# Row maxima of one main tile per head, taken for both heads together with 64-row products around the tails' products with v

## What is computed

```python
q_rot, k_rot = (rotate(q), rotate(k))
scores = scale * np.matmul(q_rot, k_rot.transpose(0, 1, 3, 2))
scores = scores - np.max(scores, axis=-1, keepdims=True)
attn = np.exp(scores)
attn = attn / (np.sum(attn, axis=-1, keepdims=True) + 1e-09)
attn_out = np.matmul(attn, v)                     # [4, 8, 576, 64], all float32
x = attn_out.transpose(0, 2, 1, 3).reshape(2304, 512)
h = x @ w_in                                      # [2304, 1024]
e = np.exp(h - h.max(-1, keepdims=True)); sm = e / (e.sum(-1, keepdims=True) + 1e-09)
solu = h * sm
ln = (solu - solu.mean(-1, keepdims=True)) / np.sqrt(solu.var(-1, keepdims=True) + 1e-06) * g_ln
out = ln @ w_out
```

## Time and profile before

| | us |
|---|---|
| median of 3 runs | 489.78 (489.76 to 490.06) |
| the profiled execution | 490.39 |
| its span, first to last instruction | 488.6 |
| PE busy | 479.5 |
| DVE busy | 362.6 |
| ACT busy | 255.4 |
| POOL busy | 179.0 |

### The profile page before, as it was taken

One profiled execution on the slowest core, in us unless ns is written; L12 is line 12 of the kernel. 1 busy time (PEld: TensorE's weight loads), 2 busy tenths in 40 slices (PEclk: granted clock), 3 DMA queues, 4 the chain that ended last, 5 costly groups with the idle time before them and its releaser, 6 DMA issues.

```text
span 488.6 us, 7547 instructions
## 1 busy us (share of the span) xinstructions
PE 479.5 (98%) x2499; PEld 402.5 (82%) x2499; DVE 362.6 (74%) x566; ACT 255.4 (52%) x383; POOL 179.0 (37%) x208
## 2 busy tenths in 40 slices
PE   7899999999999999999999999999999999999997
PEld 7677888888888888888888878888888888888885
DVE  6866877786787678677866446999998899888731
ACT  4666776777687777767777343133223222222221
POOL 6855164336435542643460012233343121122110
PEclk9999999999999999999999999999999999999999
DMA  8306454535454454545433112233333233322232
GB/s 282 95 15 171 129 166 99 171 133 162 120 147 147 117 175 125 170 99 162 138 94 97 26 46 34 48 67 85 82 70 79 36 68 68 81 55 59 61 73 89
DMA packets 101006, 50.57 MB, mean 104 GB/s; under 512 B 90280, under 2 KB 90280, under 8 KB 99048
## 3 DMA queue, kind: packets, MB, share of 16 engines
q1 hardware_dynamic: 100152, 50.00, 38.5%
q10 hardware_dynamic: 816, 0.10, 0.1%
HBM read 33.33 MB, written 4.79 MB: 78 GB/s over the span
## 4 chain that ended last, share of the span: by engine, by line
PE 92%; DMA 2%; DVE 2%; ACT 1%; POOL 1%; SPq 1%; issue 1%; POOLq 0%; DVEq 0%; ACTq 0%
PE ps L1017 24%; PE ps L1045 20%; PE ps L1031 20%; PE ps L984 17%; PE ps L955 8%; PE ps L999 4%; DMA X<-x_in 2%; POOL X L379 1%; DVE nm L735 1%; SPq L281 0%; ACT p_main L548 0%; DVE X L676 0%; DVE X L702 0%; ACT QK L504 0%; DVE X L681 0%
## 5 line engine op out<-in xcount | busy, mean ns | idle before, releaser
L735 DVE TENSOR_REDUCE nm<-ps 128x1 fp32r<-128x576 f32 x144 | 108.1, 755 | 56.8 <-PE ps L955 54.8
L1017 PE MATMUL ps<-p_main,V 128*128 128x288 f32 x512 | 145.4, 406 | 0.0
L548 ACT ACTIVATE p_main<-ps 128x576 f32<-128x576 f32 x128 | 83.2, 650 | 47.4 <-PE ps L984 45.8
L379 POOL TENSOR_TENSOR X<-X,rope 128x1152 f32<-128x1152 f32 x28 | 73.5, 2644 | 91.6 <-DVE w_lo L752 89.1
L1017 PEld LDWEIGHTS ps<-p_main,V 128*128 128x128 f32 x512 | 90.1, 190 | 13.7 <-ACT p_main L548 0.2
L984 PE MATMUL ps<-QK 128*128 128x288 f32 x320 | 95.8, 380 | 0.8 <-ACT p_main L548 0.5
L1031 PE MATMUL ps<-w_hi,KB 128*128 128x512 f32 x288 | 91.4, 390 | 0.0
L1045 PE MATMUL ps<-w_hi,QK 128*128 128x512 f32 x288 | 91.0, 389 | 0.0
L984 PEld LDWEIGHTS ps<-QK 128*128 128x128 f32 x320 | 57.6, 189 | 20.8 <-issue 5.7
L984 PE MATMUL ps<-KB 128*128 128x288 f32 x320 | 67.8, 293 | 0.0
L569 ACT ACTIVATE X<-ps,neg_max 128x1024 f32<-128x1024 f32 x18 | 20.1, 1119 | 83.1 <-DVE neg_max L773 83.1
(11 more groups left out here) (87 smaller groups left out, 574.6 us busy)
## 6 DMA issues: line engine op xcount, KB each, us to landing
X<-x_in SPq DMA_DIRECT2D x14, 1152.0 KB, 5.1
V<-oe SPq DMA_DIRECT2D x213, 32.0 KB, 1.9
V<-v_in SPq DMA_DIRECT2D x32, 160.0 KB, 2.8
out<-X SPq DMA_DIRECT2D x18, 256.0 KB, 2.3
w_raw<-w_in SPq DMA_DIRECT2D x16, 256.0 KB, 3.0
xT<-oe SPq DMA_DIRECT2D x16, 144.0 KB, 2.4
inv<-inv_rows SPq DMA_DIRECT2D x16, 144.0 KB, 3.0
xT<-oe SPq DMA_DIRECT2D x16, 128.0 KB, 2.3
```

Of the source, the lines that this page charges most:

```text
L379: nc.gpsimd.tensor_tensor(x, x, rope[:, :, :], ALU.mult).then_inc(done, 1)
L548: nc.scalar.activation(dst[:, :].rearrange("p (b c) -> p b c", b=2), score_ps[:, :, 0:HALF], ACT.Exp, scale=SCALE).then_inc(exp_done, 1)
L735: nc.vector.tensor_reduce(nm[g][:, at:at + 1], src[:, :, 0:HALF], AX_XY, ALU.max, negate=True)\
L1017: ins = nc.tensor.matmul(o_ps[a][:, half, 0:HALF], v, p[:, half * HALF:(half + 1) * HALF], start=(k == 0), stop=(k == 9))
```

## The change

For pairs `m` from 3 (`JOINT`) on, the fourth main tile of each head (tiles 3 and 8) is no longer made by two products over 128 rows. `joint_scores` makes both heads' tiles together: per half of the keys (288 of them) one product over a's 64 rows and one over b's 64 rows, into the two banks of the one place for maxima, from the high parts alone. The first half stands directly ahead of `weigh_tails` in step 5, the second directly behind it. DVE reduces each half to one value per query and head (`nm_half`), takes the smaller negated value of the two halves (`nm[2]`), and turns it (`turned[2]`). Step 6 has no maxima any more. The tail tile's maxima and b's first mains come a step earlier (`JOINT_ORDER`). `rows_of_a` and `rows_of_b` have one transfer less each, and the two rows of the joint tiles go out in `rows_of_both`, which stands in SP's list behind `load_x`. On DVE `w_low` moves from step 2 to step 1, and `add` stands between the two halves.

```diff
 STEPS = 9
+JOINT = 3
+
+JOINT_ORDER = (0, 1, 2, 4, 5, None, None, 6, 7)
...
+JOINT_MAXIMA = [((s,), (), ()) for s in range(5)] + [((5,), (), (6,)), ((), (), ()), ((7,), (), ()), ((8,), (), ())]
...
             def rows_of_a(m):
                 done = rows_early[m % 2]
                 sp.wait_ge(turned[0], m)
-                for j in range(BOTH):
+                for j in range(BOTH if m < JOINT else BOTH - 1):
                     row_part(m, 0, D, main_col(0, j), j, 4, done)
...
+            def rows_of_both(m):
+
+                sp.wait_ge(turned[2], m - JOINT + 1)
+                row_part(m, 2, D, main_col(0, BOTH - 1), 0, 4, rows_early[m % 2])
+                row_part(m, 2, 0, main_col(1, BOTH - 1), 1, 4, rows_late[m % 2])
...
                 if n + 3 < PAIRS:
                     load_x(n + 3)
+                if JOINT <= n + 1 < PAIRS:
+                    rows_of_both(n + 1)
                 if 1 <= n < PAIRS - 1:
                     inverse_out(n - 1)
...
+            def joint_max(m, k):
+
+                second = k % STEPS == BOTH + 2
+                nc.vector.tensor_reduce(nm_half[int(second)][:, :], max_slot(k)[0][:, :, 0:HALF], AX_X, ALU.max, negate=True)\
+                  .then_inc(max_taken, 1)
+                if second:
+                    dve.wait_ge(max_taken, k + 1)
...
+                    nc.vector.tensor_tensor(nm[2][:, 0:2], nm_half[0][:, :], nm_half[1][:, :], ALU.min)\
+                      .then_inc(halves_joined, 1)
+                    dve.wait_ge(halves_joined, m - JOINT + 1)
+                    nc.vector.transpose(nm_row[2][:, :], nm[2][:, :].bitcast(F32)).then_inc(turned[2], 1)
...
-                    if s == 2 and n >= 2:
+                    if s == 1 and n >= 2:
                         w_low(n - 2)
-                    if s == 5 and n + 2 < PAIRS:
-                        add(n + 2)
...
+            def joint_scores(m, k):
+
+                c, half = m % 2, k % STEPS - BOTH - 1
+                for a in range(2):
+                    at, keys = main_col(a, BOTH - 1), COLS[a] + half * HALF
+                    ins = nc.tensor.matmul(max_slot(k)[0][:, a, 0:HALF], QK[c][own(a), 0, at:at + P],
+                                           QK[c][own(a), 1, keys:keys + HALF], start=True, stop=True)
+                ins.then_inc(max_ready, 1)
```

More of the change, by code:

```diff
@@ L11 @@
 ACT = mybir.ActivationFunctionType
+AX_X = mybir.AxisListType.X
 AX_XY = mybir.AxisListType.XY
@@ L80, in attention_then_mlp @@
         rope = sb("rope", [P, 2, S])
-        nm = [sb(f"nm{g}", [P, TURN], F32R) for g in range(2)]
-        nm_row = [sb(f"nm_row{g}", [P, TURN]) for g in range(2)]
+        nm = [sb(f"nm{g}", [P, TURN], F32R) for g in range(3)]
+        nm_row = [sb(f"nm_row{g}", [P, TURN]) for g in range(3)]
+        nm_half = [sb(f"nm_half{h}", [P, 2]) for h in range(2)]
         tail_k = sb("tail_k", [P, S], F32R)
@@ L125, in attention_then_mlp @@
         max_taken = sem("max_taken")
-        turned = [sem(f"turned{g}") for g in range(2)]
+        turned = [sem(f"turned{g}") for g in range(3)]
+        joint_zero = sem("joint_zero")
+        halves_joined = sem("halves_joined")
         score_ready = sem("score_ready")
@@ L394, in set_tails @@
                 if m >= 2:
[L395 removed]
+                    pool.wait_ge(max_ready, STEPS * (m - 1) + tails_at(m - 1) + 1)
                     pool.wait_ge(tails_set, 3 * m - 3)
@@ L722, in low_queries, with row_max @@
                   .then_inc(low_q_done[a], 1)
-            def row_max(m, i):
-                k, g = STEPS * m + i, int(i > BOTH)
+            def joint_max(m, k):
[4 more added lines that the diff above has]
+                    dve.wait_ge(max_taken, k + 1)
+                    if m == JOINT:
+                        dve.wait_ge(joint_zero, 1)
+                    else:
+                        dve.wait_ge(turned[2], m - JOINT)
+                        dve.wait_ge(rows_early[(m - 1) % 2], early(m - 1))
+                        dve.wait_ge(rows_late[(m - 1) % 2], uses(m - 1) * LATE * 16)
+                    nc.vector.tensor_tensor(nm[2][:, 0:2], nm_half[0][:, :], nm_half[1][:, :], ALU.min)\
+                      .then_inc(halves_joined, 1)
+                    dve.wait_ge(halves_joined, m - JOINT + 1)
+                    nc.vector.transpose(nm_row[2][:, :], nm[2][:, :].bitcast(F32)).then_inc(turned[2], 1)
+            def row_max(m, place):
+                k, i = STEPS * m + place, tile_at(m, place)
                 dve.wait_ge(max_ready, k + 1)
+                if i is None:
+                    joint_max(m, k)
+                    return
+                g = int(i > BOTH)
                 if i == 0 and m == 1:
@@ L736, in row_max @@
                   .then_inc(max_taken, 1)
-                if (i == BOTH and m >= 1) or i == STEPS - 1:
+                if (i == BOTH and m >= 1) or place == STEPS - 1:
                     dve.wait_ge(max_taken, k + 1)
@@ L854, in _ @@
                             row_max(n + 1, i)
+                        if place == 0 and s == 5 and n + 2 < PAIRS:
+                            add(n + 2)
                     if n == 1 and s == 0:
@@ L929, in first_row, with row_scores @@
                   .then_inc(first_rows, 1)
-            def row_scores(m, i):
-                c, k = m % 2, STEPS * m + i
+            def joint_scores(m, k):
[5 more added lines that the diff above has]
+                ins.then_inc(max_ready, 1)
+            def row_scores(m, place):
+                c, k, i = m % 2, STEPS * m + place, tile_at(m, place)
                 if i == 0:
@@ L942, in row_scores @@
                     pe.wait_ge(max_taken, ahead)
+                if i is None:
+                    joint_scores(m, k)
+                    return
                 if i == BOTH and m >= 1:
```

8 lines of the change are left out of this document (7 added, 1 removed).

## The result

The changed kernel takes 501.65 us (median of 4 runs, 501.1 to 501.93), and the kernel before, on the same chip, 489.77 (489.64 to 490.06). The ratio is 1.0236 (95% interval 1.0222 to 1.025): 11.9 us slower. The forecast was 499.2, in a range of 489.5 to 503.5.

A forecast was written before the change was run, and what follows sets the result against it. PE, busy 98% of the span, bounds the kernel; changed, a loop through SP's list and the load decides. 490.39 + 9.4 (11 x 0.86) = 499.8 profiled; median 0.61 lower: 499.2 us, range 489.5 to 503.5.

The forecast's parts named there:

- The loop: From a pair's first scores over `take_o`, SP's list, the load and the rows to the next first scores: 17.69 us.
- 0.1 after the load: The joint rows, issued some 1.5 us behind the load of x, land 0.1 us after it, at 190.15.
- Rivals 1 and 2: Rows pass the load: 1, PE's own sum counts, 490.1 us; 2, DVE also keeps up, 486.7 us; chance 0.10 each.
- The price of the loop: At the pairs' borders: +0.86 us per pair in the 11 pairs with a load, 9.4 us.
- Rival 3: SP's list has a slow issue in most pairs, or the load takes longer: 504 to 510 us, chance 0.10.
- PE alone: PE's own terms per changed pair: -0.24 + 0.16 + 0.10 = +0.02 us, between -0.24 and +0.5.
- Step 6: Without its two maxima products the step falls from 1.77 to 1.53 us: -0.24 per pair.
- step 5's work: Around the tails: two halves of 0.13 us replace the old maxima's 0.27, change 0; +0.26 if products don't run at once.
- rival 4: The 64-row products of a half follow each other: +0.5 us, moves no forecast; chance 0.10.
- The wait of the second half: Behind the tails in step 5, PE waits for DVE's maximum of the first half: +0.16 us, 0 to +0.3.
- Step 3's term: Step 3's maxima wait for a maximum standing behind `w_low` on DVE: +0.10 us taken, 0 to +0.20.
- One sign: In the changed profile, the tails of pairs 13, 14 and 15 would be 16.8 us apart.

The follow-up runs named there:

- The second: The kernel before the change, with head a's fourth main tile row issued directly behind the load of x: 504.12 us against 490.18, ratio 1.0283.
- third experiment: The changed kernel with head a's joint row issued from ACT's list instead of SP's: 505.17 us, ratio 1.0305.
- the fourth: The changed kernel with 288 KB of x loaded once more directly behind the load in pairs 2 to 12: 517.2 us, ratio 1.0551.
- the first experiment: The changed kernel with the two joint rows issued ahead of the load of x in SP's list: 492.55 us against 490.18, ratio 1.0049.
- the sixth experiment: The changed kernel with joint rows ahead of the load, `w_low` in step 3 and POOL's rotations not waiting for it: 499.14 us, ratio 1.0195.

## Why the prediction came out right, and where it was off

*The loop.* It was right as drawn. Its two legs, forecast and measured in pair 10: from the first scores to the load's issue 184.93 - 172.51 = 12.42 by the prediction (its 172.62, less the weight load of 0.11) and 210.33 - 197.92 = 12.41 in the trace; from the issue to the next first weight load 190.31 - 0.11 - 184.93 = 5.27 by the prediction, and 5.20 in that pair, 5.29 as the mean of the eleven. That a row behind the load waits for the load was an inference from one small transfer. The second and third experiments confirm it, and the fourth shows that it grows with the bytes ahead, by 0.84 us for 288 KB. "0.1 after the load" holds for the bulk of the load only: in pair 3 PE resumed 4.97 us behind the issue and in pair 8 5.25, where the loads landed after 5.57 and 8.00. Rivals 1 and 2, rows that pass, are excluded.

*The price of the loop* was too small: 9.4 us forecast (11 x 0.86 is 9.5), 11.8 measured. Six of the eleven pairs took 17.38 to 17.66 us, 17.51 in the mean, which is 0.67 more than before against the 0.86 forecast. Their first leg is the forecast one, and their second is 5.14 in the mean where 5.27 was reckoned. That the load goes out 1.84 us behind the tails, where 2.05 was reckoned, saves nothing: step 3's longer wait only moves the tails towards it, and the leg from the first scores stays 12.41. The other five took 18.06 to 18.60, 18.39 in the mean. In three of them SP was late (2.50, 2.96 and 2.57 us behind the tails), in two the load took 5.7 and 5.8 us. In pair 7 it is one issue of an inverse row that took 1.34 for 0.60, and then the load stood another 0.35 without a cause that the trace names:

```profile
151.39 1.34 SPq L345 DMA_DIRECT2D inv<-inv_rows  x1
152.78 0.60 SPq L346 DMA_DIRECT2D inv<-inv_rows  x1
153.42 2.75 SPq L297 DMA_DIRECT2D KB<-nm_row  x5
156.76 0.34 SPq L268 DMA_DIRECT2D X<-x_in  x1
```

So 11 x 0.67 + 5 x 0.88 = 11.8. The term of the prediction that was mis-sized is what it left out of the forecast itself: slow issues, which it put "on top" with up to 2.9 us and which cost 2.5 in three pairs, and slow loads, for which it had 5.0 to 5.2 us and which cost 1.9 in two. One slow issue in twelve on a single line, in a list of more than a dozen, made a few hit pairs in eleven the likely case and not the bound. Rival 3 named this mechanism, for most pairs; it was five of eleven. The quick pairs were cheaper than reckoned, by 11 x 0.19 = 2.1 us, so the two errors cancelled in part, and that is luck.

*PE alone.* Step 6 was as forecast: from its scores to the next it is 1.54 us (191.40 to 192.94 in the changed kernel) where pair 15 had 1.53, and over the two steps behind the tails PE is 0.22 us quicker in the first experiment (185.69 to 188.89) than in the kernel before (184.05 to 187.47). The two products of a half do run together, so step 5's work is unchanged and rival 4 is excluded (PE before and behind pair 11's tails, for two halves of two products each):

```profile
225.86 0.40 PE L984 MATMUL ps<-QK 64*128 64x288 f32 x2
226.10 1.13 PE L1059 MATMUL ps<-p_tail,V 64*128 64x288 f32 x8
227.12 0.40 PE L984 MATMUL ps<-QK 64*128 64x288 f32 x2
227.45 0.54 PE L1044 MATMUL ps<-QK 128*128 128x288 f32 x2
```

From 225.86 to 226.10 it is 0.24: the half's 0.13 and the open weight load of 0.11, which stood ahead of the tails before and now stands ahead of the half. The 0.11 is by how much weight loads follow each other in this trace, where two of 128 rows take 0.30 us and one 0.19; nothing more stands open at the half. The wait of the second half was 0.16 to 0.17, where 0.16 was forecast: PE's loads follow the first half's products by 1.02 us (184.34 to 185.36 in the first experiment), where 1.01 was reckoned. The split to 224 keys shows its price: 2.06 / 13 = 0.16 by the medians, 0.10 to 0.14 by single pairs. Step 3's term was wrong, 0.26 where 0 to 0.20 was the bound: I carried over the 0.05 us in which PE follows a maximum from another tile's row, and for the tail tile it is 0.23. It hid in the loop and shows only in the first experiment, which came out at +2.4 us (13 x 0.18 = 2.3) instead of near 0.

*`add`.* It ran directly behind the first half's maximum, as drawn. The joint rows were turned 3.35 us behind the tails' start (193.40 - 190.05 in pair 9), where 186.5 - 182.9 = 3.6 was reckoned, and step 7's maxima did not wait.

*SP and the sign.* The chance of 0.8 for slower rested on the loop, and the loop did it alone: PE's sum, with step 3 as measured, is only +2.3 us. One sign was misread: the tails of pairs 14 and 15 could not be 16.8 us apart, since in the kernel before they are 20.8 apart already, with other work between them.

## What to carry to other kernels

When a change moves the last piece of something that the next stage needs, look at what stands ahead of it in the list of transfers: here a row of 512 bytes behind a load of 1,152 KB took about as long as the load, from either of two queues (PE resumed 5.20 and 5.44 us behind the load's issue), and exchanging two statements was worth 9.1 us. Reckon a loop that comes to bind with the spread of its slow steps, not with their usual length, because it has no slack to hide them. And before you take a wait away, ask what it keeps apart: GpSimd's wait for `w_low` looked needless, and with it dropped and `w_low` moved by two steps the kernel lost 6.6 us (499.14 against 492.55), since the two operations then ran at once and `w_low` took 3 us where it had taken 0.75.

## What the runs showed of the hardware beyond expectation

- VectorE's `w_low` took 0.69 to 0.75 us alone and 2.96 to 3.17 in 11 of 16 cases, in each of which a rotation of GpSimd (2.65 us in the median) ran beside it. In one more case the two ran at once too, and there `w_low` (at 223.18) took 0.71 and the rotation 3.16. The line (shortest, median and longest, in ns) is that of `w_low` in the sixth experiment:

```profile
L797 DVE SCALAR_TENSOR_TENSOR w_lo<-w_raw,gain,w_hi x16: 690/2970/3168, 63.2 to 308.1; 128x512 fp32r<-128x512 f32 x16
```

- A 512-byte transfer on ACT's queue, issued 1.53 us behind a large load on SP's, came no earlier than one on SP's own queue: PE resumed 5.44 and 5.20 us behind the load's issue. Issued 0.02 us ahead of the load, it came no earlier either (5.17).
- When PE had stood still for 2.3 to 2.6 us at the first scores, the granted clock then fell to 0.50 in three pairs (one of the third experiment, two of the fourth), at a cost of 1.6 us each; other waits of 2.4 and one of 3.2 us were followed by no fall.
- PE followed VectorE's maximum by 0.05 us in one place and by 0.23 in another. A distance that is read at one wait can't be carried to the next.
